# Seven block products instead of eight for the up projections of two of three token blocks, and the down products of a run in one stretch

## The chip, the cores and the metric

The kernel runs on one core of a Trainium2 chip. The metric is the time of one execution in device microseconds, the median of three runs. Five engines work side by side and meet at semaphores: TensorE (PE in the rows; PEld is its weight load), VectorE (DVE), ScalarE (ACT), GpSimd (POOL) and SyncE (SP), whose queue issues the transfers.

## What is computed

A linear attention over 1536 tokens (two sequences of 768, eight heads of 64), then four experts over all tokens, then a gated projection, all in fp32:

```python
for e in range(E):                      # E = 4, D = 512, F = 1024
    h = np.maximum(x @ w1[e], 0.0)
    out += p[:, e:e + 1] * (h @ w2[e])
...
a = x @ w1                              # second layer, 512 -> 1024
b = x @ w2
h = a * b @ w3                          # 1024 -> 1024
return (h @ w_out).astype(np.float32)   # 1024 -> 512
```

`w3 @ w_out` is folded into one 1024 x 512 matrix at the start of the program (`fold_step`), so that the second layer is two up projections, a product, and one down product.

## The kernel before

Every fp32 operand of a matmul is held as two fp32r halves, high and low (`split3`): the high half is a copy made by ScalarE, the low half is the whole minus the high half, and a product is three matmuls (high-high, high-low, low-high). A matmul here has a 128x128 stationary operand and 512 moving columns.

The program goes in stages: the fold; the attention over twelve chunks of 128 tokens (`outputs`, `scores`, `from_state`, `update`), whose result is written as `xh` and `xl`; the experts; the second layer. The experts loop over expert `e`, token block `c` (three of 512 tokens, `CW`) and tile `f` of 128 hidden columns (eight, `FT`). A step is twelve matmuls of `up` (L822) into one bank for the next `f`, and twelve of `expert_down` (L837, L838, L842) for this `f`, which add into the four banks 0 to 3 over all eight `f`. The second layer has the same loops with two `up` products a step and one down product (L891, L892, L896).

Around the matmuls: VectorE takes an up bank, applies the ReLU and the routing weight `pb` (L664) and writes `hid`; ScalarE writes its high half `hidh`; VectorE writes its low half `hidl` (the helper at L558, which subtracts two tiles in SBUF). The weights are split one 128x512 unit at a time, high on ScalarE, low on GpSimd (L447, `unit_low`, also two tiles in SBUF). After eight steps VectorE adds the four banks into `acc` (L675).

The order on each engine is the order in which the code is written. Nothing is scheduled at run time except by the semaphores.

Of the kernel before, what the change touches and what calls it, by code (L numbers as in the profile page):

```python
# [6 lines left out]
def attention_moe_projection(nc, qT, kT, k_rev, v_rev, lam, domain_probs, moe_w1, moe_w2, w1, w2, w3T, w_out, out):  # L7
# [3 lines left out]

    F32, F32R = mybir.dt.float32, mybir.dt.float32r
# [5 lines left out]
    E, FT, _, DM = moe_w1.shape  # L18
# [5 lines left out]
    KT = DM // P  # L24
    CW = 512
    NC = T // CW
    ST = CW // P
    FG = FT // 2
    RAW = 8
    NPOW = P + 1  # L30
    DOWNS = FT - 1 + KT
    BLANKS = 5


    UNITS = [("up", 0), ("up", 1)]
    for f in range(2, FT):
        UNITS += [("up", f), ("down", f - 2)]
    UNITS += [("down", FT - 2), ("down", FT - 1)]
    NU = len(UNITS)
    EARLY = NU - 2  # L40

    def unit_at(kind, f):
        return UNITS.index((kind, f))


    FIRST = {1: 0, 2: 1, 4: 2, 5: 3, 7: 4, 8: 5, 10: 6, 11: 7}

    def slot_of(g):

        return g % (RAW // 2) if g < RAW else g % RAW  # L50

    def loads_of(g):
        return sum(slot_of(j) == slot_of(g) for j in range(g + 1))

    def before(g):

        return max([j for j in range(g) if slot_of(j) == slot_of(g)], default=None)

    ctx = ExitStack()
    with ctx:  # L60
# [15 lines left out]

        x_at = region(2 * KT * T * 4)
        slab_at = region(4 * FT * CW * 4)
        fold_at = region(2 * FT * DM * 4)
        raw_at = region(RAW * CW * 4)  # L80
        pb0_at = region(CW * 4)
        misc_at = region(5440)
        work = region(0)[0]

        x_region = x_at[0]
        xh = place(x_at, "xh", [P, KT, T], F32R)
        xl = place(x_at, "xl", [P, KT, T], F32R)

        uph = place(slab_at, "uph", [P, FT, CW], F32R)
        upl = place(slab_at, "upl", [P, FT, CW], F32R)  # L90
        dnh = place(slab_at, "dnh", [P, FT, CW], F32R)
        dnl = place(slab_at, "dnl", [P, FT, CW], F32R)

        foldh = place(fold_at, "foldh", [P, FT, DM], F32R)
        foldl = place(fold_at, "foldl", [P, FT, DM], F32R)
        raw_region = raw_at[0]
        raw = place(raw_at, "raw", [P, RAW, CW])


        w_at = [x_region]  # L100
        wo_raw = place(w_at, "wo_raw", [P, FT, DM])
        w3_raw = place(w_at, "w3_raw", [P, 2, FT, CW])
        assert w_at[0] <= x_at[0]

# [84 lines left out]
        def out_bank(i):  # L189

            return ps[i % 2]
# [781 lines left out]
```

## Time and profile before

| | us |
|---|---|
| median of 3 runs | 829.05 (828.93 to 829.12) |
| the profiled execution, its own time | 828.76 |
| its span, first to last instruction | 826.9 |
| busy: PE, PEld | 819.8, 670.5 |
| busy: DVE, ACT, POOL | 272.7, 167.3, 153.8 |

The span is what the trace shows; the time of the execution has 1.9 us more around it. A matmul's busy time overlaps that of its neighbours, since matmuls are pipelined, so the pace is read from the distance between starts. A number in front of x in a row is how many instructions the row groups; "idle before" is how long the engine stood still before them, with what ended it.

### The profile page before, as it was taken

Reading aid. Unit: us, or ns where it says so; the run is one execution under the profiler, and the core shown is the slowest. Engines: PE = TensorE matmul, PEld = TensorE weight load, DVE = VectorE, ACT = ScalarE, POOL = GpSimd, SP = SyncE. Lnnn points to the kernel's source line nnn. Section 1 sums busy time; section 2 is a strip of 40 time slices with the busy share of each in tenths; the row PEclk is TensorE's granted clock in tenths of the full one; section 3 lists DMA queues with packets and bytes.
Section 4 is the critical chain, followed back from the end, with each engine's and each line's share of the span. In section 5 each row is a group of like instructions: output and inputs, shape, how many; then the busy total and the mean of one; then the engine's idle time right before and its main releaser. Section 6 shows DMA issues by size and latency. Waiting matters only on the chain.

```text
span 826.9 us, 9271 instructions
## 1 busy us (share of the span) xinstructions
PE 819.8 (99%) x3994; PEld 670.5 (81%) x3994; DVE 272.7 (33%) x415; ACT 167.3 (20%) x281; POOL 153.8 (19%) x202
## 2 busy tenths in 40 slices
PE   9999999999999999999999999999999999999998
PEld 7878888888888888888888888888888888888886
DVE  7268723233232323232323233242424112112112
ACT  7222320112211102320111221021323111111111
POOL 8636630003410002430000440000242000000000
PEclk9999999999999999999999999999999999999999
DMA  9597520002210001230000231000110001000001
GB/s 336 196 260 236 168 83 13 1 13 76 80 61 11 2 1 39 76 115 1 13 1 26 73 107 26 1 0 1 52 52 0 1 1 51 1 1 18 34 1 51
DMA packets 33544, 47.05 MB, mean 57 GB/s; under 512 B 3544, under 2 KB 13280, under 8 KB 33504
## 3 DMA queue, kind: packets, MB, share of 16 engines
q1 hardware_dynamic: 33344, 46.44, 17.6%
q8 instruction: 31, 0.51, 0.2%
q14 instruction: 9, 0.07, 0.0%
q10 hardware_dynamic: 160, 0.02, 0.0%
HBM read 43.28 MB, written 3.18 MB: 56 GB/s over the span
## 4 chain that ended last, share of the span: by engine, by line
PE 97%; DVE 1%; issue 0%; POOL 0%; ACT 0%; POOLq 0%
PE banks L822 48%; PE banks L837 11%; PE banks L838 11%; PE banks L842 11%; PE banks L735 5%; PE banks L891 3%; PE banks L896 3%; PE banks L892 3%; PE banks L747 1%; PE banks L769 1%; PE banks L777 1%; PE banks L793 1%; PE banks L785 0%; DVE probs L599 0%; DVE fin L710 0%
## 5 line engine op out<-in xcount | busy, mean ns | idle before, releaser
L822 PE MATMUL banks<-xh,uph 128*128 128x512 f32 x480 | 189.6, 395 | 0.0
L822 PE MATMUL banks<-xh,upl 128*128 128x512 f32 x480 | 188.7, 393 | 0.0
L822 PE MATMUL banks<-xl,uph 128*128 128x512 f32 x480 | 187.1, 390 | 0.0
L478 ACT ACTIVATE hidh<-hid 128x512 fp32r<-128x512 f32 x120 | 75.9, 632 | 488.9 <-DVE hid L664 422.5
L664 DVE SCALAR_TENSOR_TENSOR hid<-banks,pb 128x512 f32<-128x512 f32 x96 | 66.3, 690 | 294.3 <-PE banks L822 294.3
L837 PE MATMUL banks<-hidh,dnh 128*128 128x512 f32 x384 | 151.1, 394 | 0.0
L838 PE MATMUL banks<-hidh,dnl 128*128 128x512 f32 x384 | 150.8, 393 | 0.0
L447 POOL TENSOR_TENSOR upl<-raw,uph 128x512 fp32r<-128x512 f32 x40 | 52.2, 1304 | 420.5 <-ACT uph L478 420.5
L558 DVE TENSOR_TENSOR hidl<-hid,hidh 128x512 fp32r<-128x512 f32 x120 | 83.5, 696 | 83.7 <-ACT hidh L478 83.7
L822 PEld LDWEIGHTS banks<-xh,upl 128*128 128x128 f32 x480 | 90.1, 188 | 21.5
L822 PEld LDWEIGHTS banks<-xl,uph 128*128 128x128 f32 x480 | 90.2, 188 | 20.9
L822 PEld LDWEIGHTS banks<-xh,uph 128*128 128x128 f32 x480 | 90.1, 188 | 19.3
L842 PE MATMUL banks<-hidl,dnh 128*128 128x512 f32 x384 | 103.6, 392 | 0.0
L838 PEld LDWEIGHTS banks<-hidh,dnl 128*128 128x128 f32 x384 | 72.1, 188 | 16.5
L837 PEld LDWEIGHTS banks<-hidh,dnh 128*128 128x128 f32 x384 | 72.0, 188 | 16.3
L842 PEld LDWEIGHTS banks<-hidl,dnh 128*128 128x128 f32 x384 | 72.1, 188 | 16.0
L703 DVE TENSOR_TENSOR hid<-banks,first 128x512 f32<-128x512 f32 x24 | 16.6, 691 | 132.0 <-PE banks L822 132.0
L447 POOL TENSOR_TENSOR dnl<-raw,dnh 128x512 fp32r<-128x512 f32 x40 | 52.5, 1314 | 36.2 <-ACT dnh L478 36.2
L822 PE MATMUL banks<-xh,dnh 128*128 128x512 f32 x96 | 37.4, 389 | 0.0
L822 PE MATMUL banks<-xl,dnh 128*128 128x512 f32 x96 | 37.4, 389 | 0.0
L822 PE MATMUL banks<-xh,dnl 128*128 128x512 f32 x96 | 37.4, 389 | 0.0
L891 PE MATMUL banks<-foldh,hidh 128*128 128x512 f32 x92 | 36.6, 398 | 0.0
(105 smaller groups left out, 636.8 us busy)
## 6 DMA issues: line engine op xcount, KB each, us to landing
raw<-in_moe_w SPq DMA_DIRECT2D x64, 256.0 KB, 2.8
w_raw<-in_w3T SPq DMA_DIRECT2D x16, 256.0 KB, 6.5
raw<-in_w SPq DMA_DIRECT2D x16, 256.0 KB, 2.8
pb<-route_scratch SPq DMA_DIRECT2D x12, 256.0 KB, 3.5
out<-fin SPq DMA_DIRECT2D x12, 256.0 KB, 2.1
wo_raw<-in_w_out SPq DMA_DIRECT2D x8, 256.0 KB, 5.4
over_xh<-in_kT SPq DMA_DIRECT2D x4, 256.0 KB, 6.1
over_xh<-in_q SPq DMA_DIRECT2D x4, 256.0 KB, 5.8
```

What stands on the lines that cost most here:

```text
L447: tt(lo[:, f, :], raw[:, slot_of(g), :], hi[:, f, :].bitcast(F32), ALU.subtract).then_inc(unit_lo, 1)
L478: return nc.scalar.activation(dst, src, ACT.Copy)
L558: sub = lambda dst, whole, high: nc.vector.tensor_tensor(dst, whole, high.bitcast(F32), ALU.subtract)
L664: nc.vector.scalar_tensor_tensor(out=hid[:, f % 2, :], in0=up_bank(f), scalar=0.0, in1=pb[c], op0=ALU.max, op1=ALU.mult).then_inc(hid_read ...
L735: last = mm(fold_bank(row), x, y, start=c == 0 and i == 0, stop=c == FT - 1 and i == 2)
L822: last = mm(bank, x, y, start=kt == 0 and i == 0, stop=kt == KT - 1 and i == 2)
L837: mm(ps[d], dnh[:, f, ds], hidh[:, f % 2, :], start=f == 0, stop=False)
L838: mm(ps[d], dnl[:, f, ds], hidh[:, f % 2, :], start=False, stop=False)
L842: last = mm(ps[d], dnh[:, f, ds], hidl[:, f % 2, :], start=False, stop=f == FT - 1)
L891: mm(ps[t], hidh[:, f % 2, ts], foldh[:, f, :], start=f == 0, stop=False)
L892: mm(ps[t], hidh[:, f % 2, ts], foldl[:, f, :], start=False, stop=False)
L896: last = mm(ps[t], hidl[:, f % 2, ts], foldh[:, f, :], start=False, stop=f == FT - 1)
```

## The change

Two neighbouring tiles of hidden columns are now made together in a "run" `w`: 256 hidden columns for all three token blocks. There are 16 runs for the experts (four for each) and 8 for the second layer (a run for w1 and one for w2, four times). For token blocks 0 and 1 the product of the 2x2 blocks is made as seven block products in place of eight (`product`, six matmuls each: P1 to P7) from sums of blocks of the weights (`sums`, GpSimd) and of the tokens (`T1` to `T4`, VectorE), put together again by five sums on VectorE (`sum_u2`, `sum_u3`, `sum_c22`, `sum_c21`, `sum_c12`). Token block 2 is made as before (`third`, Ua and Ub, twelve matmuls each). A run gives six hidden tiles in the order `ORDER`.

The down products of a run are twelve groups of six matmuls (`group`), one for each token block and 128 output columns, each added into `acc` by VectorE (`add_group`). They stand in one stretch behind P1 of the next run; a second-layer run for w2 has none, the last twelve stand at the end, and before run 16 eight of them come ahead of P1. In the expert runs the low halves of the hidden tiles are made by GpSimd (`hidden_low`) and no longer by VectorE, in a ring of three tiles; in the runs for w2 they are made by VectorE. GpSimd also makes the low halves of the weights (`a_low`, `s_low`) for the next run and of the down weights (`d_low`), 128x1024 at a time. The folded matrix goes through DRAM and comes back as a down weight. The attention's ends change: the first eight chunks are written to `acc` and split from there.

```diff
+    NQ = E * FG
+    RUNS = NQ + 2 * FG
+    GR = KT * NC
+    OUTS = 6
+    A11, A12, A21, A22, S3, S4, S1, S2 = range(8)
+    B11, B21, B22, T1, T2, T3, T4 = range(7)
+    PIECES = ("P1", "P6", "P5", "P2", "P7", "Ua", "P4", "P3", "Ub")
+
+    ORDER = (0, 3, 4, 1, 2, 5)
...
@@ -461,15 +507,92 @@
-                if i in FIRST:
-                    unit_low(FIRST[i])
-            for e in range(E):
-                for c in range(NC):
-                    for f in range(FT):
-                        for g in splits_at(e, c, f):
-                            unit_low(g)
-            for f in range(2):
-                unit_low(E * NU + EARLY + f)
...
+            def a_low(j):
+                s = j % 2
+                pool.wait_ge(wa_hi, j + 1)
+                low(w_l[s][:, A11:A22 + 1, :], up_src(j), w_h[s][:, A11:A22 + 1, :]).then_inc(wa_lo, 1)
+
...
+            def s_low(j):
+                s = j % 2
+                pool.wait_ge(ws_hi, j + 1)
+                low(w_l[s][:, S3:S2 + 1, :], up_src(j), w_h[s][:, S3:S2 + 1, :]).then_inc(ws_lo, 1)
+
+            def d_low(j):
+                pool.wait_ge(wd_hi, j + 1)
+                low(d_l[j % 2][:, :, :], dn_raw[j % 2][:, :, :], d_h[j % 2][:, :, :]).then_inc(wd_lo, 1)
+
+            def hidden_low(n):
+                j = ORDER[n % OUTS]
+                pool.wait_ge(h_hi, n + 1)
+                low(hl[:, j, :], ring_at(n), hh[:, j, :]).then_inc(h_lo, 1)
+
+            for w in range(NQ):
+                later = 2 <= w + 1
+                if later:
+                    a_low(w + 1)
+                    sums(w + 1)
+                hidden_low(OUTS * w)
+                if later:
+                    s_low(w + 1)
+                hidden_low(OUTS * w + 1)
+                d_low(w)
+                for k in range(2, OUTS):
+                    hidden_low(OUTS * w + k)
+
...
+            def snapshot(w):
+                act.wait_ge(piece_done, made(w, "P1"))
+                if w > 0:
+                    act.wait_ge(c21_ready, w)
+                copy(v1[:, :], bank_x).then_inc(v1_ready, 1)
+
+            def hidden_high(n):
+                Q, k = divmod(n, OUTS)
+                c = ORDER[k] // 2
+                act.wait_ge(r_ready, n + 1)
+                if Q > 0:
+
+                    act.wait_ge(group_done, GR * (Q - 1) + KT * (c + 1))
+                copy(hh[:, ORDER[k], :], ring_at(n)).then_inc(h_hi, 1)
+
+            for w in range(NQ):
+                later = 2 <= w + 1
+                snapshot(w)
+                if later:
+                    a_high(w + 1)
+                hidden_high(OUTS * w)
+                if later:
+                    s_high(w + 1)
+                hidden_high(OUTS * w + 1)
+                d_high(w)
+                for k in range(2, OUTS):
+                    hidden_high(OUTS * w + k)
...
+            def sum_c22(w, dst):
+                dve.wait_ge(piece_done, made(w, "P5"))
+                dve.wait_ge(u3_ready, w + 1)
+                tt(dst, u3[:, :], bank_z, ALU.add).then_inc(c22_ready, 1)
+
+            def sum_c21(w, dst):
+                dve.wait_ge(piece_done, made(w, "P4"))
+                tt(dst, v1[:, :], bank_y, ALU.add).then_inc(c21_ready, 1)
+
+            def sum_c12(w, dst):
+                dve.wait_ge(piece_done, made(w, "P3"))
+                dve.wait_ge(u2_ready, w + 1)
+                tt(dst, u2[:, :], bank_z, ALU.add).then_inc(c12_ready, 1)
+
+            def gate(n, src):
+
+                j = ORDER[n % OUTS]
+                nc.vector.scalar_tensor_tensor(out=ring_at(n), in0=src, scalar=0.0, in1=pb[:, j // 2, :],
+                                               op0=ALU.max, op1=ALU.mult).then_inc(r_ready, 1)
+
+            def ring_free(n):
+
+                if n >= OUTS * NQ:
+                    dve.wait_ge(h_lo, n - 1)
+                elif n >= 3:
+                    dve.wait_ge(h_lo, n - 2)
+
...
+            for w in range(NQ):
+                e, q = divmod(w, FG)
+                n = OUTS * w
+                add_groups(w - 1, range(GR))
+                sum_u2(w)
+                if w == 0:
+                    t3_low(0)
...
+                dve.wait_ge(piece_done, made(w, "P2"))
+                ring_free(n)
+                gate(n, bank_x)
+                sum_u3(w)
+                ring_free(n + 1)
+                sum_c22(w, ring_at(n + 1))
+                dve.wait_ge(c22_ready, w + 1)
+                gate(n + 1, ring_at(n + 1))
+                dve.wait_ge(piece_done, made(w, "Ua"))
+                ring_free(n + 2)
+                gate(n + 2, bank_x)
+                ring_free(n + 3)
+                sum_c21(w, ring_at(n + 3))
+                dve.wait_ge(c21_ready, w + 1)
+                gate(n + 3, ring_at(n + 3))
+                ring_free(n + 4)
+                sum_c12(w, ring_at(n + 4))
+                dve.wait_ge(c12_ready, w + 1)
+                gate(n + 4, ring_at(n + 4))
+                dve.wait_ge(piece_done, made(w, "Ub"))
+                ring_free(n + 5)
+                gate(n + 5, bank_y)
...
+            for w in range(NQ, RUNS):
+                Q = hidden_of(w)
+                else:
+                    sum_u2(w)
+                    dve.wait_ge(piece_done, made(w, "P2"))
+                    dve.wait_ge(a_copied, 3 * (Q - NQ) + 1)
+                    ring_free(n)
+                    times(n, bank_x, a_tile[ORDER[0]])
...
+                    dve.wait_ge(c22_ready, w + 1)
+                    times(n + 1, ring_at(n + 1), a_tile[ORDER[1]])
+                    hidden_low(n)
+                    dve.wait_ge(piece_done, made(w, "Ua"))
+                    dve.wait_ge(a_copied, 3 * (Q - NQ) + 2)
+                    ring_free(n + 2)
+                    times(n + 2, bank_x, a_tile[ORDER[2]])
+                    hidden_low(n + 1)
+                    ring_free(n + 3)
+                    sum_c21(w, ring_at(n + 3))
...
+            def product(bank, s, a, b, start):
+                for k in range(KH):
+                    ks = slice(k * P, (k + 1) * P)
+                    for i, (x, y) in enumerate(split3((w_h[s][:, a, ks], w_l[s][:, a, ks]),
+                                                      (xs_h[:, b, k, :], xs_l[:, b, k, :]))):
+                        last = mm(bank, x, y, start=start and k == 0 and i == 0, stop=k == KH - 1 and i == 2,
+                                  skip_group_check=True)
+                last.then_inc(piece_done, 1)
...
-            def expert_down(e, c, f):
-                at = e * (NC * FT) + c * FT + f
-                if c == 0:
-                    pe.wait_ge(unit_lo, e * NU + unit_at("down", f) + 1)
-                pe.wait_ge(hid_hi, at + 1)
-                for d in range(KT):
-                    if f == 0:
-                        pe.wait_ge(bank_left, e * (NC * KT) + c * KT + d + 1)
-                    ds = slice(d * P, (d + 1) * P)
-                    mm(ps[d], dnh[:, f, ds], hidh[:, f % 2, :], start=f == 0, stop=False)
-                    mm(ps[d], dnl[:, f, ds], hidh[:, f % 2, :], start=False, stop=False)
-                pe.wait_ge(hid_lo, at + 1)
-                for d in range(KT):
-                    ds = slice(d * P, (d + 1) * P)
-                    last = mm(ps[d], dnh[:, f, ds], hidl[:, f % 2, :], start=False, stop=f == FT - 1)
-                    if f == FT - 1:
-                        last.then_inc(down_done, 1)
-                if f < FT - 1:
-                    last.then_inc(down_done, 1)
-
+                last.then_inc(piece_done, 1)
+
+            def group(g):
+                Q, at = divmod(g, GR)
+                c, s = at // KT, Q % 2
+                pe.wait_ge(wd_lo, Q + 1)
+                pe.wait_ge(h_lo, OUTS * Q + 4 + c)
+                if g >= 5:
+                    pe.wait_ge(acc_done, g - 4)
+                ds = slice(at % KT * P, (at % KT + 1) * P)
+                for u in range(2):
+                    if Q < NQ:
+                        pairs = split3((d_h[s][:, u, ds], d_l[s][:, u, ds]), (hh[:, 2 * c + u, :], hl[:, 2 * c + u, :]))
                     else:
-                        output(c, f)
+                        pairs = split3((hh[:, 2 * c + u, ds], hl[:, 2 * c + u, ds]), (d_h[s][:, u, :], d_l[s][:, u, :]))
+                    for i, (x, y) in enumerate(pairs):
+                        last = mm(group_bank(g), x, y, start=u == 0 and i == 0, stop=u == 1 and i == 2)
+                last.then_inc(group_done, 1)
...
+                if w == NQ:
+                    groups(old, range(0, 2 * KT))
+                product(bank_x, s, A11, B11, True)
+                groups(old, range(GR) if w != NQ else range(2 * KT, GR))
...
+                product(bank_y, s, S2, T2, True)
...
+                product(bank_z, s, S1, T1, True)
+                pe.wait_ge(v1_ready, w + 1)
...
+                product(bank_x, s, A12, B21, False)
+                pe.wait_ge(u2_ready, w + 1)
...
+                product(bank_y, s, S3, T3, False)
...
+                third(bank_x, s, A11)
+                pe.wait_ge(u3_ready, w + 1)
...
+                product(bank_y, s, A22, T4, False)
+                pe.wait_ge(c22_ready, w + 1)
...
+                product(bank_z, s, S4, B22, False)
+                pe.wait_ge(c21_ready, w + 1)
+                third(bank_y, s, A21)
+
+            for w in range(RUNS):
+                run(w)
+            groups(NQ + FG - 1, range(GR))
```

How the rows move on the engines. On POOL, in the middle of the experts, before (`upl`, `dnl` are low halves of up and down weights, `raw` the loaded unit):

```order
133 L447 TENSOR_TENSOR dnl<-raw,dnh 128x512 [waits unit_hi]
134 L447 TENSOR_TENSOR upl<-raw,uph 128x512 [waits unit_hi]
135 L447 TENSOR_TENSOR dnl<-raw,dnh 128x512 [waits unit_hi]
136 L447 TENSOR_TENSOR upl<-raw,uph 128x512 [waits unit_hi]
137 L447 TENSOR_TENSOR dnl<-raw,dnh 128x512 [waits unit_hi]
```

and of the change, one run (`w_l` is the low half of four weight blocks, `hl` of a hidden tile, `d_l` of the down weights, `up_raw` the loaded blocks, which the sums overwrite):

```order
172 L493 TENSOR_TENSOR w_l_55<-up_raw_68,w_h_54 128x1024 [waits wa_hi]
173 L542 TENSOR_TENSOR up_raw_68<-up_raw_68 128x256 [waits wa_lo]
174 L544 TENSOR_TENSOR up_raw_68<-up_raw_68 128x256 [waits ws_sum]
175 L546 TENSOR_TENSOR up_raw_68<-up_raw_68 128x256 [waits ws_sum]
176 L548 TENSOR_TENSOR up_raw_68<-up_raw_68 128x256 [waits ws_sum]
177 L493 TENSOR_TENSOR hl<-ring,hh 128x512 [waits h_hi]
178 L493 TENSOR_TENSOR w_l_55<-up_raw_68,w_h_54 128x1024 [waits ws_hi]
179 L493 TENSOR_TENSOR hl<-ring,hh 128x512 [waits h_hi]
180 L493 TENSOR_TENSOR d_l_61<-dn_raw_71,d_h_60 128x1024 [waits wd_hi]
181 L493 TENSOR_TENSOR hl<-ring,hh 128x512 [waits h_hi] x4
```

Between the first hidden tile of a run and its last four, POOL's queue now has two instructions of 128x1024, one for the next run's weights and one for this run's down weights.

On DVE, two steps of the experts before:

```order
157 L558 TENSOR_TENSOR hidl<-hid,hidh 128x512 [waits hid_hi]
158 L664 SCALAR_TENSOR_TENSOR hid<-banks,pb_65 128x512 [waits up_done]
159 L558 TENSOR_TENSOR hidl<-hid,hidh 128x512 [waits hid_hi]
160 L664 SCALAR_TENSOR_TENSOR hid<-banks,pb_65 128x512 [waits up_done]
161 L558 TENSOR_TENSOR hidl<-hid,hidh 128x512 [waits hid_hi]
```

and of the change, one run from its first sum (`banks` is PSUM, `v`, `u` and `ring` are SBUF tiles):

```order
242 L908 TENSOR_TENSOR u_66<-v_65,banks 128x512 [waits c12_ready,v1_ready,piece_done]
243 L933 SCALAR_TENSOR_TENSOR ring<-banks,pb 128x512 [waits h_lo,piece_done]
244 L914 TENSOR_TENSOR u_67<-v_65,banks 128x512 [waits c22_ready,piece_done]
245 L919 TENSOR_TENSOR ring<-u_67,banks 128x512 [waits u3_ready,piece_done,h_lo]
246 L933 SCALAR_TENSOR_TENSOR ring<-ring,pb 128x512 [waits c22_ready]
247 L933 SCALAR_TENSOR_TENSOR ring<-banks,pb 128x512 [waits h_lo,piece_done]
248 L923 TENSOR_TENSOR ring<-v_65,banks 128x512 [waits piece_done,h_lo]
249 L933 SCALAR_TENSOR_TENSOR ring<-ring,pb 128x512 [waits c21_ready]
250 L928 TENSOR_TENSOR ring<-u_66,banks 128x512 [waits u2_ready,piece_done,h_lo]
251 L933 SCALAR_TENSOR_TENSOR ring<-ring,pb 128x512 [waits c12_ready]
252 L933 SCALAR_TENSOR_TENSOR ring<-banks,pb 128x512 [waits h_lo,piece_done]
253 L959 TENSOR_TENSOR acc<-banks,acc 128x512 [waits group_done] x12
```

The subtractions for the hidden tiles are gone from this engine, and three of the six gates (rows 246, 249, 251) now read both their inputs from SBUF.

## Rows read from the trace of the kernel before

**Rows 1.** The page: engines, slices with the clock, chain of waits.
```profile
PE 819.8 (99%) x3994; PEld 670.5 (81%) x3994; DVE 272.7 (33%) x415; ACT 167.3 (20%) x281; POOL 153.8 (19%) x202
...
PEclk9999999999999999999999999999999999999999
...
PE 97%; DVE 1%; issue 0%; POOL 0%; ACT 0%; POOLq 0%
```

**Rows 2.** Timeline of PE, VectorE, ScalarE: one step of the experts (start, length, us).
```profile
301.42 0.40 PE L822 MATMUL banks<-xh,uph 128*128 128x512 f32 x1
...
303.96 0.39 PE L822 MATMUL banks<-xh,upl 128*128 128x512 f32 x1
304.19 0.40 PE L837 MATMUL banks<-hidh,dnh 128*128 128x512 f32 x1
...
304.39 0.69 DVE L664 SCALAR_TENSOR_TENSOR hid<-banks,pb 128x512 f32<-128x512 f32 x1 [3.46 <-PE banks L822]
...
305.12 0.63 ACT L478 ACTIVATE hidh<-hid 128x512 fp32r<-128x512 f32 x1 [4.90 <-DVE hid L664]
...
305.78 0.69 DVE L558 TENSOR_TENSOR hidl<-hid,hidh 128x512 fp32r<-128x512 f32 x1 [0.70 <-ACT hidh L478]
...
306.95 0.40 PE L822 MATMUL banks<-xh,uph 128*128 128x512 f32 x1
```

**Rows 3.** Timeline: the first matmuls of the experts, and two pairs in the second layer.
```profile
93.92 0.48 PE L822 MATMUL banks<-xh,uph 128*128 128x512 f32 x1
94.23 0.40 PE L822 MATMUL banks<-xl,uph 128*128 128x512 f32 x1
...
702.00 0.39 PE L822 MATMUL banks<-xh,dnl 128*128 128x512 f32 x1
702.23 0.40 PE L891 MATMUL banks<-foldh,hidh 128*128 128x512 f32 x1
702.47 0.39 PE L892 MATMUL banks<-foldl,hidh 128*128 128x512 f32 x1
```

**Rows 4.** Groups of instructions by line, shapes apart: count, busy us, mean ns.
```profile
L447 POOL TENSOR_TENSOR dnl<-raw,dnh 128x512 fp32r<-128x512 f32 x40 | 52.5, 1314 | 36.2 <-ACT dnh L478 36.2
L425 POOL TENSOR_TENSOR prods<-prods 8x192 f32<-8x192 f32 x1 | 0.6, 588 | 0.1
L423 POOL TENSOR_TENSOR prods<-prods,prod 8x64 f32<-8x64 f32 x1 | 0.3, 311 | 0.1
L478 ACT ACTIVATE hidh<-hid 128x512 fp32r<-128x512 f32 x120 | 75.9, 632 | 488.9 <-DVE hid L664 422.5 <-DVE hid L703 66.5
L675 DVE TENSOR_TENSOR acc<-banks,acc 128x512 f32<-128x512 f32 x36 | 22.4, 682 | 5.5 <-PE banks L842 5.5
```

**Rows 5.** Timeline of VectorE and GpSimd where their work overlaps.
```profile
53.69 1.06 POOL L456 TENSOR_TENSOR k_dec<-chunk_b,decay 128x512 f32<-128x512 f32 x1 [9.49 <-PE banks L785]
53.72 1.57 DVE L609 TENSOR_TENSOR qs<-chunk_b,q_pow 128x512 f32<-128x512 f32 x1
...
112.68 2.55 POOL L447 TENSOR_TENSOR dnl<-raw,dnh 128x512 fp32r<-128x512 f32 x2 [2.98 <-ACT dnh L478]
...
184.61 1.30 POOL L447 TENSOR_TENSOR upl<-raw,uph 128x512 fp32r<-128x512 f32 x1 [69.38 <-ACT uph L478]
...
631.15 1.68 POOL L447 TENSOR_TENSOR dnl<-raw,dnh 128x512 fp32r<-128x512 f32 x1 [6.85 <-ACT dnh L478]
631.61 1.77 DVE L558 TENSOR_TENSOR xl<-acc,xh 128x512 fp32r<-128x512 f32 x1
632.79 1.75 POOL L447 TENSOR_TENSOR dnl<-raw,dnh 128x512 fp32r<-128x512 f32 x1
```

**Rows 6.** Stretches: fold and attention, experts, second layer. Busy us and count, clock.
```profile
0.00:93.90 93.90, 90.00 (x826) 75.72 (x827) 60.15 (x102) 31.34 (x51) 59.12 (x129) 1.00 0.77 248
93.90:625.00 531.10, 531.10 (x2307) 432.60 (x2306) 165.74 (x245) 103.16 (x176) 91.25 (x71) 1.00 0.13 39
625.00:823.60 198.60, 198.60 (x866) 162.22 (x864) 46.00 (x67) 32.78 (x54) 3.39 (x2) 1.00 0.03 12
```

More of the change, by code:

```diff
@@ L27, in attention_moe_projection, with made @@
     ST = CW // P
-    FG = FT // 2
-    RAW = 8
+    FT = 2 * FG
     NPOW = P + 1
-    DOWNS = FT - 1 + KT
     BLANKS = 5
[L35 to L57, printed above, removed]
+    BW = KH * P
+    NQ = E * FG
[6 more added lines that the diff above has]
+    ORDER = (0, 3, 4, 1, 2, 5)
+    def made(w, piece):
+        return len(PIECES) * w + PIECES.index(piece) + 1
     ctx = ExitStack()
@@ L376, in _ @@
[L376 to L379 removed]
+            load_chunk(4)
+            load_chunk(5)
+            for row in range(FG, FT):
+                store_fold(row)
+            for i in range(PLACES, NCH):
+                load_chunk(i)
+            sp.wait_ge(attended, NCH)
@@ L380, in _ @@
+            for t in range(NC * ST):
+                sp.wait_ge(acc_done, GR * (NQ + FG - 1) + t + 1)
+                sp.dma_start(out[t * P:(t + 1) * P, :], outs[:, t, :]).then_inc(out_done, 16)
             sp.wait_ge(out_done, 16 * NC * ST)
@@ new lines, in _ @@
+            for w in range(NQ):
[10 more added lines that the diff above has]
+                    hidden_low(OUTS * w + k)
+            for which, rows in ((B11, slice(0, KH)), (B21, slice(KH, KT))):
+                for k in range(KH):
+                    pool.wait_ge(b_hi, NB + 1 + (which == B21))
+                    low(xs_l[:, which, k, :], acc[:, rows.start + k, 0:CW], xs_h[:, which, k, :]).then_inc(b_lo, 1)
@@ new lines, in _ @@
+            t_low(1, T1, t1)
+            t_low(1, T2, T2_AT)
+            for k in range(KH):
+                pool.wait_ge(b_hi, NB + 3)
+                low(xs_l[:, B22, k, :], acc[:, KH + k, CW:2 * CW], xs_h[:, B22, k, :]).then_inc(b_lo, 1)
+            t_low(1, T4, T4_AT)
+            for w in range(NQ, RUNS):
+                if w + 1 < RUNS:
+                    a_low(w + 1)
+                    sums(w + 1)
+                    s_low(w + 1)
+                if first(w):
+                    d_low(hidden_of(w))
@@ new lines, in _, with b_high @@
+            for w in range(NQ):
[10 more added lines that the diff above has]
+                    hidden_high(OUTS * w + k)
+            def b_high(which, rows, cols, group):
+                act.wait_ge(acc_done, group)
+                copy(xs_h[:, which, :, :], acc[:, rows, cols]).then_inc(b_hi, 1)
@@ L633, in _ @@
             mask(0)
-            for row in range(FG, FT):
-                fold_low(row)
             for i in range(NCH):
```

900 lines of the change are left out of this document (530 added, 370 removed).

## Prediction, on record before the change was timed

> **What bounds the kernel now.** I read the page first: TensorE is busy for 99% of the span at the full granted clock (2.4 GHz), and the chain of waits lies on it for 97% [rows 1]. The windows say the same of each stage from the experts on: 531.10 us of 531.10, then 198.60 of 198.60 [rows 6]. So the time is a count of matmuls times their pace, and any new TensorE wait is paid in full. The timeline gives the pace: one expert step of 24 matmuls goes from 301.42 to 306.95 [rows 2], 5.53 us, 0.2304 us each. It also gives the hand-overs. VectorE starts 0.43 us after the start of the last matmul it waits for (303.96 to 304.39), which is 0.20 us after the next matmul could start. Its 0.69 us end at 305.08 and ScalarE starts at 305.12; ScalarE ends at 305.75 and VectorE starts at 305.78 [rows 2]. I take 0.04 us for each hand-over.
>
> **What the change removes.** For two of three token blocks, eight products of six matmuls become seven. That is 6 matmuls for each of 24 runs, 144 in all, of 3168 behind the attention. At 0.2304 us they are worth **33.2 us**. The down products keep their count: 20 hidden runs by 12 groups by 6. The pace itself has bounds. Two matmuls of one second-layer bank start 0.23 us apart and a pair with a bank change 0.24 (702.00, 702.23, 702.47) [rows 3]. I keep 0.2304; 1% either way on 3024 matmuls is 7 us.
>
> **What it adds: the tail of an expert run.** TensorE must not reach the down groups before GpSimd has made four low halves (`group` waits for `h_lo` 6Q+4). I count from the end of P2 (t = 0). Then come P7, Ua, P4, P3, Ub and the next P1, 48 matmuls, so without waits the groups would start at 48 x 0.2304 = 11.06. Durations: VectorE 0.69, ScalarE 0.63 at 512 columns [rows 2, 4]. GpSimd takes 1.26 from start to start at 512 columns (two instructions in 2.55) [rows 5]. At 1024 columns no row shows either engine. GpSimd took 0.31 at 64 and 0.59 at 192 columns, 2.2 ns a column, which agrees with 1.31 at 512 [rows 4]; so 1024 costs about 2.4, between that and twice 1.26. ScalarE lies between 0.63 and 1.26; I take 1.17, because most of its time should grow with the columns.
>
> Without interference: gate 0 on VectorE 0.20 to 0.89, ScalarE to 1.56, first low half on GpSimd to 2.87. Behind it in GpSimd's queue stand `s_low` (2.4), low half 1 (1.26), `d_low` (2.4), low halves 2 and 3 (2.5): the fourth is ready at 11.4, TensorE waits 0.4.
>
> But there is interference. At 53.72 VectorE starts a product of two SBUF tiles 0.03 us behind a GpSimd instruction and needs 1.57 us instead of 0.69: it ends 0.54 after GpSimd's. At 631.61 one that starts inside a GpSimd instruction (631.15 to 632.83) needs 1.77, and the GpSimd instruction behind it takes 1.75 instead of 1.30 [rows 5]. A VectorE instruction with two SBUF inputs waits until the running GpSimd instruction is over, then takes 0.55, and delays the next one by 0.43. The sums and gates that read PSUM are free of it: 0.68 at acc<-banks,acc [rows 4]. The Trainium skill, page "SBUF — State Buffer", section "Who interferes with whom", states it as a rule: a VectorE instruction with two SBUF inputs and a GpSimd one that reads SBUF lock each other out for the whole instruction. By that rule, the trace agrees. The rule speaks against this change: with it the sum below is a loss, without it a gain of some 20 us.
>
> Three gates of a run (1, 3, 4) now read two SBUF tiles while GpSimd works without a pause. With the lock:
> P7 is done at 1.58 for VectorE; u3 to 2.27, c22 to 2.99, gate 1 at 3.03. GpSimd began `s_low` at 2.87 and holds until 5.27; gate 1 ends 5.8. ScalarE to 6.5, low half 1 to 7.8. Gate 2 to 6.5, c21 to 7.15: Ub waited for it since 6.92, so TensorE waits **0.3**. Gate 3 waits for low half 1 and ends 8.35; `d_low` (7.8, plus 2.4, plus 0.43) ends 10.6. c12 to 9.0; gate 4 waits for `d_low`, ends 11.2. Low half 2, delayed by 0.43, ends 12.3, low half 3 at 13.55. TensorE ends P1 at 11.06 + 0.3 = 11.4 and waits until about 13.65: **2.3**. Together 2.6 us a run. The chain restarts with every P2, and GpSimd catches up in the 16.6 us of the groups. Runs 1 to 14 pay it: 14 x 2.6 = **36.4 us**.
>
> **The other terms.** Run 0 has no `s_low`: 0.5. Behind run 15 eight groups come ahead of P1, which no longer covers: 3.9. Run 16 needs new token sums made from the last experts' output. VectorE's sums and low halves meet twelve GpSimd instructions of 1.26, and P6 (waits for `tp_lo` 10) and Ua (waits for the third block's low halves, queued ahead of u3) each come some 1.5 late: 3, between 0 and 6. In a w2 run there are no groups. `s_high` holds ScalarE until 4.5 (`a_low` and four sums of about 0.7 end at 3.3), `s_low` then holds VectorE's second low half until 7.45, c21 comes at 8.1 and not before 6.92: 1.25 in three runs and 0.2 in the last, 4. In the attention VectorE gains two sums of 1024 columns, lying where it is already busy 60 of 94 us [rows 6], and loses one 0.69 subtraction in each of eight chunks; P2 and P7 of run 0 wait some 0.5 each for the last sums: 1.5, between 0 and 4. A matmul behind a wait is followed after 0.31 us and not 0.23 (93.92, 94.23) [rows 3]: 0.08 at some 30 waits, 2. The extra transfers (the folded matrix out and back, 512 KB loads) are asked for a run or more ahead on a queue whose engines work 13% of the time [rows 6]: nothing. If a load were late, it would cost its lateness in every run. The end stays: last bank, one VectorE instruction, one transfer.
>
> **Sum**: -33.2 + 36.4 + 0.5 + 3.9 + 3 + 4 + 1.5 + 2 = +18.1 us. The profiled execution's 828.76 becomes 846.9; the median of the runs is 0.3 above it, so **847 us**, from 841 (pace 1% better) to 853 (pace 1% worse, or GpSimd 2.55 at 1024 columns, 0.3 a run).
>
> **Rivals.**
> 1. *The lock is small here, the change pays.* The gates are another operation than those in the rows (scalar_tensor_tensor reading two SBUF tiles; every one of its 96 before reads PSUM). If they aren't held up, a run costs 0.4, the passage to run 16 3, the w2 runs 0.5, the start 1, restarts 1.5, run 0 0.4: -33.2 + 6 + 6.4 = 808 us. Against it: the rows show the lock for two operands in SBUF whatever is multiplied. The change pays as long as the wait stays under (33.2 - 15) / 14 = 1.3 us a run. Chance 0.33, with everything between 803 and 827.
> 2. *Gate 1 gets in ahead of `s_low`.* They come 0.16 us apart (3.03 and 2.87). Then gate 1 ends 3.7, low half 1 at 6.95, `d_low` at 9.8, low half 3 at 12.7: the wait is 1.7 a run, c21 is in time. 829 - 33.2 + 24 + 14 = 834 us. Chance 0.13. Together with what falls between it and no gain, within 0.2% of before: 0.04.
> 3. *More than the lock.* The stops of over 2 us in each run let the granted clock fall, or GpSimd's 1024 columns cost 2.6 and more: above 853. For it: the trace of before has no TensorE stop as long, so it shows nothing of the clock behind one. Chance 0.05.
> 4. *Forecast*: the lock as worked out, 841 to 853. Chance 0.45.
>
> So faster by over 0.2% (what a measurement of this kernel can tell from no change) has 0.33, within it 0.04, slower 0.63 (the forecast, rivals 2 and 3). Own range of the forecast: 841 to 853. The range that holds the time 8 times in 10 has to take in most of the first rival: 806 to 853.
>
> **What the profile of the changed kernel would show.** Right: 3850 matmul records or a few less; TensorE idle time of some 2.3 us a run ahead of the first down group, released by GpSimd's low half, and 0.3 ahead of Ub, released by VectorE; VectorE's gates from SBUF to SBUF over 1.2 us in the mean with the first some 2.8; GpSimd's 512-column low halves from 1.3 to 1.7. Rival 1: those gates at 0.7. Rival 2: a short first gate and a stretched `s_low`. The sum fails if the matmul pace is far from 0.2304 in the stretches without waits, if a load or the routing weights come late, or if VectorE falls behind the groups (0.69 in every 1.38 us).

## The result

| | before | after |
|---|---|---|
| median of the timed runs, us | 829.02 (828.93 to 829.12) | 856.36 (849.61 to 862.10) |
| ratio, with its 95% interval | | 1.0327 (1.0250 to 1.0403) |
| the profiled execution, its own time | 828.76 | 849.61 |
| its span | 826.9 | 847.8 |

The change makes the kernel slower by 3.3%. The forecast was 847 with 806 to 853 as its range. The direction is as forecast and the median lies above the range. One thing about the kernel is new: its four executions differ by 12.5 us where those of before differ by 0.2. Their mean granted clocks were 0.996, 0.980, 0.986 and 0.988 in the order of the times 849.61, 862.10, 857.25 and 855.47. The profiled one is the fastest, and it alone lies in the forecast's own range of 841 to 853.

The page of the changed kernel, with the engines, the clock in 40 slices, the chain of waits, the low halves of hidden tiles and the gates between SBUF tiles (these answer to [rows 1, 4]):

```profile
PE 788.9 (93%) x3850; PEld 641.5 (76%) x3850; DVE 500.2 (59%) x617; ACT 204.4 (24%) x292; POOL 444.5 (52%) x396
...
PEclk9999999999999999999999999999999899999999
...
PE 82%; DVE 11%; issue 5%; POOL 1%; ACT 0%; DMA 0%; DVEq 0%
...
L493 POOL TENSOR_TENSOR hl<-ring,hh 128x512 fp32r<-128x512 f32 x96 | 128.9, 1363 | 234.1 <-ACT hh L601 234.1
...
L493 POOL TENSOR_TENSOR w_l<-up_raw,w_h 128x1024 fp32r<-128x1024 f32 x44 | 105.9, 2406 | 88.4 <-ACT w_h L601 88.4
...
L933 DVE SCALAR_TENSOR_TENSOR ring<-ring,pb 128x512 f32<-128x512 f32 x48 | 98.1, 2043 | 1.6
...
L933 DVE SCALAR_TENSOR_TENSOR ring<-banks,pb 128x512 f32<-128x512 f32 x48 | 32.9, 686 | 50.1 <-PE banks L1178 31.1
```

TensorE is busy for 93% and no longer 99%, with 144 matmuls fewer. The same gate takes 686 ns when it reads its bank and 2043 ns in the mean when it reads two SBUF tiles. One slice shows a clock under full.

The timeline of one steady run, first VectorE, then GpSimd (start, length, engine, line), as in [rows 5]:

```profile
308.31 0.69 DVE L919 TENSOR_TENSOR ring<-u,banks 128x512 f32<-128x512 f32 x1
309.03 2.73 DVE L933 SCALAR_TENSOR_TENSOR ring<-ring,pb 128x512 f32<-128x512 f32 x1
311.68 0.68 DVE L933 SCALAR_TENSOR_TENSOR ring<-banks,pb 128x512 f32<-128x512 f32 x1
312.29 0.67 DVE L923 TENSOR_TENSOR ring<-v,banks 128x512 f32<-128x512 f32 x1
312.99 1.35 DVE L933 SCALAR_TENSOR_TENSOR ring<-ring,pb 128x512 f32<-128x512 f32 x1
314.26 0.67 DVE L928 TENSOR_TENSOR ring<-u,banks 128x512 f32<-128x512 f32 x1
314.97 2.17 DVE L933 SCALAR_TENSOR_TENSOR ring<-ring,pb 128x512 f32<-128x512 f32 x1
318.37 0.69 DVE L933 SCALAR_TENSOR_TENSOR ring<-banks,pb 128x512 f32<-128x512 f32 x1 [1.23 <-POOL hl L493]
```

```profile
307.56 1.30 POOL L493 TENSOR_TENSOR hl<-ring,hh 128x512 fp32r<-128x512 f32 x1 [14.12 <-ACT hh L601]
308.81 2.40 POOL L493 TENSOR_TENSOR w_l<-up_raw,w_h 128x1024 fp32r<-128x1024 f32 x1
312.50 1.28 POOL L493 TENSOR_TENSOR hl<-ring,hh 128x512 fp32r<-128x512 f32 x1 [1.29 <-ACT hh L601]
313.74 2.85 POOL L493 TENSOR_TENSOR d_l<-dn_raw,d_h 128x1024 fp32r<-128x1024 f32 x1
316.55 2.94 POOL L493 TENSOR_TENSOR hl<-ring,hh 128x512 fp32r<-128x512 f32 x2
```

The first of the three gates starts 0.22 us behind `s_low` and ends 0.55 after it. The second waits for a low half, the third for `d_low`. The last low half that the groups need is thus late: it ends at 319.49 (316.55 plus 2.94). TensorE's timeline shows its wait: it stands from about 317.2 to 319.59, 2.37 us more than one matmul's distance. The view does not name the releaser; the restart lies 0.10 us behind the end of that low half.

```profile
319.59 0.47 PE L1205 MATMUL banks<-hh,d_h 128*128 128x512 f32 x1 [2.21 <-issue]
319.90 0.40 PE L1205 MATMUL banks<-hl,d_h 128*128 128x512 f32 x1
320.13 0.39 PE L1205 MATMUL banks<-hh,d_l 128*128 128x512 f32 x1
```

In this execution the distances between matmul starts beyond one matmul's 0.227 add up as follows: 14 times 2.37 ahead of the groups and 0.3 or 0.5 ahead of Ub in each of these runs and in run 15; 3.70 behind run 15; 2.76 ahead of P6 and 4.63 ahead of Ua in run 16; 3 times 1.50 ahead of Ub in the w2 runs and 0.47 ahead of the last twelve groups; 0.81, 0.56 and 0.83 in run 0. Together that is 56.4 us. In the kernel before, no distance from the first expert matmul on is over 0.31.

### The profile page after: what moved, and what is told of

The parts are those of the page before. It is cut to its first block, busy times and chain, and to the rows that moved or that the text cites. A ratio compares the mean times of both kernels' runs of the same rounds, so it can differ in the third digit from the quotient of the medians.

```text
span 847.8 us, 9958 instructions
## 1 busy us (share of the span) xinstructions
PE 788.9 (93%) x3850; PEld 641.5 (76%) x3850; DVE 500.2 (59%) x617; ACT 204.4 (24%) x292; POOL 444.5 (52%) x396
## 4 chain that ended last, share of the span: by engine, by line
PE 82%; DVE 11%; issue 5%; POOL 1%; ACT 0%; DMA 0%; DVEq 0%
PE banks L1205 38%; PE banks L1178 22%; PE banks L1188 14%; PE banks L1091 5%; DVE ring L933 2%; DVE ring L923 1%; DVE xc_l L771 1%; DVE hl L771 1%; PE banks L1103 1%; PE banks L1135 1%; PE banks L1127 1%; POOL hl L493 1%; DVE qs L833 1%; POOL d_l L493 1%; DVE probs L823 1%
## 5 line engine op out<-in xcount | busy, mean ns | idle before, releaser
L493 POOL TENSOR_TENSOR hl<-ring,hh 128x512 fp32r<-128x512 f32 x96 | 128.9, 1363 | 234.1 <-ACT hh L601 234.1
L959 DVE TENSOR_TENSOR acc<-banks,acc 128x512 f32<-128x512 f32 x216 | 149.0, 691 | 161.4 <-PE banks L1205 161.4
L1205 PE MATMUL banks<-hh,d_h 128*128 128x512 f32 x384 | 150.7, 393 | 35.1 <-issue 34.4
L493 POOL TENSOR_TENSOR w_l<-up_raw,w_h 128x1024 fp32r<-128x1024 f32 x44 | 105.9, 2406 | 88.4 <-ACT w_h L601 88.4
L1205 PE MATMUL banks<-hh,d_l 128*128 128x512 f32 x384 | 149.5, 389 | 0.0
L1205 PE MATMUL banks<-hl,d_h 128*128 128x512 f32 x384 | 149.5, 389 | 0.0
L1178 PE MATMUL banks<-xs_h,w_h 128*128 128x512 f32 x336 | 131.1, 390 | 3.6 <-POOL xs_l L493 2.6
L1178 PE MATMUL banks<-xs_l,w_h 128*128 128x512 f32 x336 | 130.7, 389 | 0.0
L1178 PE MATMUL banks<-xs_h,w_l 128*128 128x512 f32 x336 | 130.7, 389 | 0.0
L933 DVE SCALAR_TENSOR_TENSOR ring<-ring,pb 128x512 f32<-128x512 f32 x48 | 98.1, 2043 | 1.6
```

The source lines that it names most:

```text
L493: return tt(dst, whole, high.bitcast(F32), ALU.subtract)
L933: nc.vector.scalar_tensor_tensor(out=ring_at(n), in0=src, scalar=0.0, in1=pb[:, j // 2, :], op0=ALU.max, op1=ALU.mult).then_inc(r_ready, 1)
L959: tt(cols, group_bank(g), cols, ALU.add).then_inc(acc_done, 1)
L1178: last = mm(bank, x, y, start=start and k == 0 and i == 0, stop=k == KH - 1 and i == 2, skip_group_check=True)
L1205: last = mm(group_bank(g), x, y, start=u == 0 and i == 0, stop=u == 1 and i == 2)
```

## The experiments

A theory and three rivals were put to the chip. **Lock**: gates with two SBUF inputs and GpSimd's instructions hold each other up, in the order in which they stand. **Amount**: GpSimd simply has too much to do ahead of the groups. **Clock**: what lies above the forecast is TensorE at its lower level behind the waits. **Pace**: matmuls are slower all through the new kernel. Each kernel ran four times beside the kernel before, whose median was 828.88 to 829.21 in the sets.

**The same kernel again.** No edit.

> The changed kernel itself, to see how its time goes with the granted clock. The profiled execution had clock 0.996 and 849.6 us; three others had 0.980 to 0.988 and 855 to 862. Theory L (the lock between VectorE and GpSimd makes 2.66 us of TensorE waiting a run, and in some executions the clock falls behind these waits): the time again lies between 849 and 862 and falls in line with the clock, some 0.8 us for 0.001. Rival P (the clock is a chance of the chip and has nothing to do with the kernel): the kernel before would scatter alike, and it did not (828.9 to 829.1).

Measured 855.16 us (851.98 to 862.05), ratio 1.0321 (1.0261 to 1.0381), clocks 0.984, 0.994, 0.980, 0.992. The profiled execution took 857.52, 7.9 more than the one above, with waits of the same length. TensorE's timeline behind one of its 2.36 us waits:

```profile
493.84 0.77 PE L1205 MATMUL banks<-hh,d_h 128*128 128x512 f32 x1 [2.20 <-issue]
494.40 0.63 PE L1205 MATMUL banks<-hl,d_h 128*128 128x512 f32 x1
494.83 0.63 PE L1205 MATMUL banks<-hh,d_l 128*128 128x512 f32 x1
...
496.54 0.63 PE L1205 MATMUL banks<-hh,d_h 128*128 128x512 f32 x1
496.96 0.44 PE L1205 MATMUL banks<-hl,d_h 128*128 128x512 f32 x1
497.25 0.39 PE L1205 MATMUL banks<-hh,d_l 128*128 128x512 f32 x1
```

Starts lie 0.43 us apart and not 0.23, some seven or eight times, then the old pace is back. The windows over a stretch of it (busy time and count of PE, PEld, DVE, ACT, POOL, then the granted clock, the share of DMA, GB/s):

```profile
420.00:440.00 20.00, 17.77 (x78) 14.39 (x78) 9.66 (x13) 2.69 (x4) 11.52 (x10) 1.00 0.09 27
...
480.00:500.00 20.00, 17.67 (x71) 13.88 (x70) 12.46 (x13) 7.01 (x10) 16.75 (x11) 0.91 0.27 92
```

That is the lower level, 1.2 GHz, for a part of the second window. It came behind 5 of the 14 waits of that length here and behind none in the fast execution. A sixth stretch at the lower level, at the end of the attention (90.9 to 94.3), cost next to nothing: the first expert matmul starts 0.27 us later, and the wait ahead of P6 in run 0 is 0.5 shorter. From the last matmul ahead of the first of these waits to the last one ahead of the next Ub it is 31.26 us with a fall (145.72 to 176.98) and 29.68 without (145.93 to 175.61): **1.6 us for each fall**. Five of them are 7.9 us, which is the whole difference between the two executions. The times 855.47, 857.25 and 862.10 lie 3.7, 4.8 and 7.9 such falls above 849.61; that is an estimate, since these executions have no trace. Pace is out as the rival for the extra, since the waits and the distances outside the falls (0.227) are the same.

**The large instructions ahead of the hidden tiles.** In runs 1 to 15, on GpSimd and on ScalarE:

```diff
-                hidden_low(OUTS * w)
                 if later:
                     s_low(w + 1)
+                    d_low(w)
+                hidden_low(OUTS * w)
                 hidden_low(OUTS * w + 1)
-                d_low(w)
```

> s_low of the next run and d_low of this run go ahead of the first hidden tile, in runs 1 to 15; ScalarE's halves of them go with it. Nothing is left out. Theory L: GpSimd holds the lock no longer than 1.3 us at a time in the tail, and four low halves are ready before P1 ends. The wait of 2.37 us ahead of the down groups goes to 0 to 0.3, that of 0.29 ahead of Ub goes too: 14 x 2.4 = 34 us less and 3 less into run 16, about 812 us, clock 1.00 in the experts and little scatter. Rival Q (GpSimd's own queue is too long, lock or not): the same 812, this run does not tell the two apart. Rival R (the new place makes the low halves late for P6 or collides with a_low): over 830.

Measured 805.22 us (805.08 to 805.35), ratio 0.9713 (0.9699 to 0.9728). Nothing is taken away, neither an instruction nor a column, and the kernel is 51 us faster than 856.36 (50 than the 855.16 beside it). All of the waits ahead of Ub and of the groups in runs 1 to 14 are gone. What is left adds up to 15.2 us, all of it outside these runs. So the amount of work on GpSimd is no cause; the place of the long instructions is. Whether they hurt there through the lock or through their own length in the queue, this run alone does not tell. The time came out 7 us under the 812 expected: that sum had left out the waits ahead of Ub (4.8 in 15 runs) and the longer distance behind each wait (0.31 and not 0.227, 2.6 in all).

**Sums kept in PSUM.** The order stays, and the three gates read a bank:

```diff
-                sum_c22(w, ring_at(n + 1))
+                sum_c22(w, ps[3])
-                gate(n + 1, ring_at(n + 1))
+                gate(n + 1, ps[3])
...
-                sum_c21(w, ring_at(n + 3))
+                sum_c21(w, ps[4])
...
-                sum_c12(w, ring_at(n + 4))
+                sum_c12(w, bank_z)
...
+                elif w <= NQ:
+                    pe.wait_ge(r_ready, OUTS * w - 1)
```

The last two lines make TensorE wait until the gate has read the bank before it writes there again.

> The order of the change stays. In the expert runs the three sums c22, c21, c12 are written to PSUM and the gates read them there, so that no VectorE instruction of the tail reads two SBUF tiles. Theory L: gates of 0.69 us instead of 2.73, 1.35 and 2.17; the wait a run goes from 2.66 to the 0.4 worked out without the lock: 849.6 - 14 x 2.25 - 2 = 816 us. Rival Q (GpSimd's own queue makes the wait: 2.4 + 2.4 + 4 x 1.3 us, lock or not): the wait stays over 2 us, 845 us or more. Rival S (a sum into PSUM is itself slower than into SBUF): gates short but the sums over 0.8 us.

Measured 816.67 us (816.34 to 819.00), ratio 0.9857 (0.9843 to 0.9872). VectorE and GpSimd in one run:

```profile
296.44 0.70 DVE L919 TENSOR_TENSOR banks<-u,banks 128x512 f32<-128x512 f32 x1
297.17 0.69 DVE L933 SCALAR_TENSOR_TENSOR ring<-banks,pb 128x512 f32<-128x512 f32 x1
```

```profile
296.94 2.42 POOL L493 TENSOR_TENSOR w_l<-up_raw,w_h 128x1024 fp32r<-128x1024 f32 x1
```

The gate starts inside the 1024-column instruction, 0.23 us behind its start (0.22 in the change), and needs 0.69 in place of 2.73. The wait ahead of the groups is 0.62 to 0.82 and none is left ahead of Ub. The time is the 816 expected, and both rivals are out: GpSimd's queue is as long as it was, and the sum into PSUM takes 0.70. This isolates the lock: the same instructions in the same order, with one input of each of three gates moved out of SBUF. What the queue costs without the lock is the 0.62 to 0.82 (0.4 in the prediction's working).

**One of the two moved.** `d_low` alone ahead of the first hidden tile, and `s_low` alone:

```diff
+                d_low(w)             (d_early)
                 hidden_low(OUTS * w)
                 s_low(w + 1)
                 hidden_low(OUTS * w + 1)
-                d_low(w)
...
+                s_low(w + 1)         (s_early)
                 hidden_low(OUTS * w)
-                s_low(w + 1)
                 hidden_low(OUTS * w + 1)
                 d_low(w)
```

> Only d_low (and ScalarE's half of it) goes ahead of the first hidden tile; s_low stays behind it. By the lock, step by step: gate 1 still waits for s_low and ends 5.8 us after P2, low half 1 at 7.9, gate 3 at 8.4 (Ub still 0.29 late), low half 2 at 9.5 held back by gate 3, gate 4 at 10.1, low half 3 at 11.2, and P1 ends at 11.2: a wait of 0.3 to 0.5 a run in all, 810 to 812 us. Rival (the two long instructions cost alike, half of the effect each): half of the 44 us between the change and order_both, about 828.

> Only s_low goes ahead of the first hidden tile; d_low stays in the tail. By the lock: gate 1 undisturbed to 3.8 us after P2, low half 1 at 5.8, d_low from 5.8 to 8.2 holds gate 3 until 8.8, low half 2 at 9.9, gate 4 at 10.4, low half 3 at 11.6 against the end of P1 at 10.9: no wait at Ub, 0.7 ahead of the groups in runs 1 to 14, about 815 us. Rival (half of the effect each): about 828.

Measured 815.66 us (815.30 to 816.71; ratio 0.9839, 0.9824 to 0.9853) and 820.93 us (820.05 to 822.00; ratio 0.9901, 0.9886 to 0.9915). Both are 4 to 6 us above what was expected, and both are well under the 828 of the rival that gives each instruction half of the effect. With `d_low` early the wait ahead of the groups is down to 0.07 and the one ahead of Ub stays, 0.29 in most runs and 0.47 in some: `s_low` still holds the first gate. With `s_low` early Ub waits for nothing and the groups wait 0.8 (once 1.16). So the two do not add up: moving either one alone takes away most of the 2.37. Against order_both, the two runs also wait longer behind run 15 (1.40 and 2.14 in place of 0.67), and in d_early the 0.07 and the longer distance behind each wait (0.31 to 0.34) come to 3.6 us, where order_both has 1.1. The expectations had neither.

**A longer wait.** One more subtraction of 1024 columns ahead of the fourth low half on GpSimd in runs 1 to 14, into a tile that nothing reads then:

```diff
                 for k in range(2, OUTS):
+                    if k == 3 and 1 <= w < NQ - 1:
+                        low(t1[...], same.bitcast(F32), same)
                     hidden_low(OUTS * w + k)
```

> One more GpSimd subtraction of 1024 columns into an unused tile, ahead of the fourth hidden tile's low half in runs 1 to 14; the output stays the same. The wait ahead of the down groups grows by 2.4 us to 4.8. Theory C (the granted clock falls behind long TensorE waits): the clock of the experts falls below 1.00 in every execution, and the time grows by more than the 14 x 2.4 = 34 us of the waits, to 890 or more. Rival P (the clock has nothing to do with the waits): 849.6 + 34 = 884 with a clock of 0.98 to 1.00 as before.

Measured 896.96 us (896.36 to 897.32), ratio 1.0819 (1.0803 to 1.0835), clock 0.969 in all four. TensorE now waits 4.2 us in each of the 14 runs, 1.85 more than before, which is 26 us. The kernel is 47.3 us above the fastest execution of the change. The other 21 us are the clock: matmuls 0.43 apart behind every one of the 14 waits, 1.5 us for each. So the clock is tied to the wait. It falls behind each wait of 4.2 us and behind a part of those of 2.37, and the spread of times goes away with the chance in it. The length of the wait does not settle it alone: the profiled executions of the change, of its repetition and of long_wait have a wait of 3.70 behind run 15 with no fall behind it, and that of psum_gates, the slowest of its four at 819.00, has a fall behind one of 1.98 and another behind 2.76.

**The w2 runs and the passage.** `order_late_s` is order_both with ScalarE's `s_high` behind its six hidden tiles in the w2 runs:

```diff
-                    hidden_high(n)
+                    for k in range(OUTS):
+                        hidden_high(n + k)
                     if w + 1 < RUNS:
                         s_high(w + 1)
-                    for k in range(1, OUTS):
-                        hidden_high(n + k)
```

> order_both, and in the runs for w2 ScalarE makes its half of s_low behind the six hidden tiles, so that GpSimd is idle while VectorE makes the low halves. By the lock the wait of 1.49 us ahead of Ub in three w2 runs goes: 805.2 - 4.5 = 800.8 us. Rival (c21 is late there because VectorE has too much to do, lock or not): 805.

Measured 800.19 us (798.52 to 801.34), ratio 0.9647 (0.9631 to 0.9663): the three waits of 1.50 are gone. The agreement with 800.8 has some chance in it: run 16 is the same code as in order_both, and its wait ahead of Ua is 3.00 here and 4.62 there, while the experts start 1.0 later. `order_trans` goes on from it: ahead of run 16 GpSimd waits until the third block's low halves are made, and makes T4 ahead of B22.

```diff
+            pool.wait_ge(xc_lo, 2 * ST)
+            t_low(1, T4, T4_AT)
             for k in range(KH):
                 pool.wait_ge(b_hi, NB + 3)
                 low(xs_l[:, B22, k, :], ...)
-            t_low(1, T4, T4_AT)
```

> order_late_s, and at run 16 GpSimd makes the low halves of T4 and then B22 only when VectorE's four low halves of the third token block are done. By the lock the 4.6 us wait ahead of Ua in run 16 goes, and with it the fall of the granted clock that follows it in every profile so far (about 1 us); P6 of run 17 waits some 1 us for s_low instead: 800.8 - 4.5 = 796 us, and the clock is 1.00 over the whole span. Rival (the wait only moves to P4 and P3 of run 16): 800.

Measured 799.86 us (799.10 to 801.79), ratio 0.9650 (0.9635 to 0.9664). The four subtractions, which took 7.03 us of VectorE between GpSimd's, took 2.49, and the wait ahead of Ua (3.00) was gone; but one of 3.81 stood behind Ub in its place, and the clock fell behind it, so that the expected 1.00 over the whole span failed too. ScalarE's timeline says why:

```profile
607.82 0.60 ACT L605 ACTIVATE a_pb<-banks 128x512 f32<-128x512 f32 x1 [2.65 <-PE banks L1184]
618.87 1.06 ACT L605 ACTIVATE w_h<-up_raw 128x1024 fp32r<-128x1024 f32 x1 [10.45 <-POOL up_raw L548]
619.83 1.04 ACT L605 ACTIVATE d_h<-dn_raw 128x1024 fp32r<-128x1024 f32 x1
620.78 0.58 ACT L605 ACTIVATE a_left<-banks 128x512 f32<-128x512 f32 x1
```

The copy of Ua's bank, which the next P1 waits for, is queued behind two instructions, the first of which waits for GpSimd, and GpSimd had just lost 5 us to the new wait. The expectation of 796 had priced the wait taken away and not the queue behind it. `passage` mends both: the low half of run 17's blocks goes into GpSimd's gap, and ScalarE copies Ua's bank first.

```diff
+            a_low(NQ + 1)
             pool.wait_ge(xc_lo, 2 * ST)
...
                         copy(a_tile[tile], bank).then_inc(a_copied, 1)
+                        if w == NQ and piece == "Ua":
+                            s_high(w + 1)
+                            d_high(hidden_of(w))
```

> The passage to the second layer, from order_trans (799.86 us, where TensorE waited 2.74 ahead of P6 of run 16, nothing ahead of Ua, and 3.81 behind Ub). In that trace GpSimd stood idle for 4.99 us (603.2 to 608.2) and ScalarE had the high half of run 17's sums, at 618.87, queued ahead of the copy of Ua's bank that the next product waits for. Here GpSimd makes the low half of run 17's four blocks in that gap, and ScalarE copies Ua's bank first. The 3.81 should fall to about 1 (GpSimd's four sums and the two halves behind them end near 620 and P6 of run 17 needs them at 619): 796 to 798 us. Rival: the 1024-column low half holds VectorE's xc_l subtractions by the lock and Ua waits some 2 us in its place: 799 to 801, no gain.

Measured **797.26 us** (797.22 to 797.46), ratio 0.9616 (0.9600 to 0.9632), the fastest here, 3.8% under the kernel before and inside the 796 to 798 expected. 2.76 us ahead of P6 are the longest wait that is left, and the clock falls behind it; behind Ub it is 1.13.

**Order and PSUM together.** order_late_s with the sums in PSUM as well:

> The kernel with every large instruction ahead of the first hidden tile or behind the last one (order_late_s, 800.19 us, whose trace has no TensorE wait of 0.2 us between run 1 and the groups behind run 15), and the three sums of a run kept in PSUM as well, so that no gate reads two SBUF tiles. The lock is then gone and not only hidden. If the lock's whole price was in the waits that it caused ahead of the down groups, there is nothing left to win: 800 us (798.5 to 801.5). Rival: the lock also costs pace that the list of waits does not show, then under 798. Second rival: three more VectorE writes into PSUM a run get in TensorE's way, then above 803.

Measured 799.16 us (797.67 to 799.73), ratio 0.9635 (0.9621 to 0.9650). That is the 800 expected; the 1 us between the medians is less than either spread. From the first expert matmul to the end of the wait ahead of P6 of run 16 the traces take 506.4 us and 508.1, and two waits that are gone (0.82 in run 0, 0.67 behind run 15) are 1.5 of the 1.6. So in the steady runs, where the order hides the lock, taking it away brings nothing: it costs only through what waits behind it.

## Why the prediction was right, and where it failed

The **mechanism and its size in a steady run** were right. Forecast were 0.3 ahead of Ub and 2.3 ahead of the groups, 36.4 us in 14 runs; the trace has 0.3 to 0.5 and 2.37, some 38 us. The experiment that takes the lock away gains what it was said to cost: 849.6 (the execution without falls in these runs) minus 816.7 is 33, and the working has 2.6 a run with the lock and 0.4 without, 31 in 14 runs. order_both, which takes it out of the way, gains 44: 37.7 in waits of runs 1 to 14, 3.3 in run 15 (no wait ahead of Ub, 3.70 to 0.67 behind it) and the rest mostly in the distances behind the waits. The three gates are held up in the order of the working, by `s_low`, by a low half, by `d_low`. Rival 1, that another operation than those of [rows 5] might not be held, is out: the gate ends 0.55 after GpSimd's instruction, as the subtraction in [rows 5] ended 0.54 after. The Trainium skill, page "SBUF — State Buffer", section "Who interferes with whom", also says that a VectorE instruction with at most one SBUF input, outside the modes that use both ports, does not contend with GpSimd; the trace agrees, 0.69 us beside a running 2.42 in psum_gates. Rival 2 is out too: gate 1 started 0.22 behind `s_low`.

**The step that failed is rival 3**, "the stops of over 2 us in each run let the granted clock fall", which the prediction put at 0.05 because no row of before has such a stop, and left out of the sum. It is true, and in the median execution it decides: at 1.6 us a fall the median of 856.36 holds about four in the steady runs (an estimate, as above), 6.8 us above 849.61. Without them the time was 849.6, 2.7 above the forecast and in its range. [Rows 1] show full clock in every slice, but of a kernel that never stops TensorE for long: that is no evidence for one that does, and deserved a bound of its own of 14 times some price, not a chance of 0.05. GpSimd's 1024 columns, the other half of that rival, took 2.40 as forecast.

The terms of the sum against the profiled execution of 849.61 (20.9 above 828.76):

| term | forecast | measured |
|---|---|---|
| matmuls taken away, and their pace | -33.2 | -42.9 |
| the longer distances behind waits | 2 | 3.6 |
| runs 1 to 14 | 36.4 | 37.7 |
| run 0 and the start | 0.5 + 1.5 | 0.8 + 2.9 |
| behind run 15 | 3.9 | 4.0 |
| run 16 | 3 | 7.4 |
| lower clock behind its second wait | 0 | 2.3 |
| w2 runs, with the last groups | 4 | 5.0 |

That this sum lands 2.7 from the forecast is in part luck: terms that were too small by some 12 us in all meet a pace that gave back 10.

- **Pace.** From the first expert matmul to the last, with the waits, the distances behind them and the slow stretch taken out, a matmul takes 0.2270 us (686.4 us for 3024) against 0.2302 before (729.3 for 3168). That is 1.4% less, beyond the bound of 1% that the prediction gave it. No run here shows why.
- **Run 16** was mis-sized: 2.76 ahead of P6 and 4.63 ahead of Ua, where 1.5 and 1.5 were said. Both lie in the work of VectorE with two SBUF inputs and up to 1024 columns between GpSimd's instructions. For the second, order_trans shows the lock as the cause (7.03 us of VectorE became 2.49); the first is 2.74 to 2.76 in every run here and was not tested. Behind the second the clock fell in this execution: twelve distances are 0.38 to 0.56.

```profile
658.26 0.76 PE L1188 MATMUL banks<-xc_h,w_h 128*128 128x512 f32 x1 [4.47 <-DVE xc_l L771]
658.82 0.63 PE L1188 MATMUL banks<-xc_l,w_h 128*128 128x512 f32 x1
659.25 0.63 PE L1188 MATMUL banks<-xc_h,w_l 128*128 128x512 f32 x1
```

The windows of the changed kernel:

```profile
600.00:620.00 20.00, 20.00 (x89) 16.55 (x89) 11.29 (x14) 1.82 (x3) 4.97 (x4) 1.00 0.00 1
...
640.00:660.00 20.00, 12.93 (x53) 10.13 (x52) 19.37 (x15) 8.24 (x11) 19.75 (x12) 0.91 0.00 1
660.00:680.00 20.00, 20.00 (x82) 16.34 (x82) 6.51 (x10) 7.17 (x10) 12.18 (x10) 0.91 0.09 27
```

- **Loads and weights** never came late, and VectorE kept up with the groups (0.69 in 1.36 us), as said.

What stays open: why the clock falls behind one wait of 2.37 us and not behind the next of the same length, with the same work around both. The spread of order_late_s (2.8 us) goes with its clock at the two ends, 0.998 at 798.52 and 0.991 at 801.34, but no trace of these two executions shows where it fell.

## What to carry to other kernels

When an engine's work is given to another, look at what both read at the same time: three gates of 0.69 us became 2.04 in the mean, because their inputs moved to SBUF while GpSimd worked without a pause. Before GpSimd's long instructions are blamed for their amount, try their order: putting 2.40 us instructions ahead of a chain that TensorE waits for, and not between its links, was worth 44 us here against the execution without falls and 51 against the median, with nothing taken away. And price a TensorE wait of some 2 us or more with more than its length, and expect executions to spread.

## What was not expected of the hardware

- The granted clock fell to 1.2 GHz behind 5 of 14 waits of 2.37 us in one execution, behind none in another, and behind all 14 of 4.2 us. It fell behind one of 1.98 us in another kernel, and behind none of three of 3.70. In the expert runs a fall was some eight matmuls 0.43 us apart, 1.5 to 1.6 us.
- scalar_tensor_tensor with two SBUF inputs is held for the whole of a GpSimd instruction: 2.73 us behind one of 2.40. GpSimd's next instruction that met a held gate took 2.85 in place of 2.40, 0.45 more, as one of 512 columns took 0.43 more.
- ScalarE needs 1.04 us for a copy of 1024 columns and 0.63 for 512; GpSimd 2.40 and 1.26. Both had been bounded only.
